# The expert jobs on TensorE: one two-way branch in place of two tests, and a prefetch hint for the narrow variant's closing jump

## The reference

```
q_n, k_n = rmsnorm(q, g_q), rmsnorm(k, g_k)            # q, k, v: 4 x 12 heads x 448 x 64
x = softmax(q_n k_n^T / 8) v                           # as rows: 1792 tokens x 768
logits = (x / |x|) (emb / |emb|)^T / tau               # 8 experts
e = argmax(logits);  gate = softmax(logits)[e]
x = gate * (relu(x @ w1[e]) @ w2[e])                   # w1[e]: 768 x 1024, w2[e]: 1024 x 768
out = (sigmoid(x @ w_gate) * (x @ w_val)) @ w_out      # 768 x 1536, 1536 x 768
```

## Time and profile before

| | us |
|---|---|
| median of three runs | 1142.76 |
| the profiled execution's own time | 1139.64 |
| span of its profile | 1138.2 |
| TensorE busy with matmuls | 1104.6 (97%) |
| TensorE weight loads | 979.2 (86%) |
| VectorE | 775.7 (68%) |
| ScalarE | 599.8 (53%) |
| GpSimd | 367.2 (32%) |

### The profile page before, as it was taken

One profiled execution on the slowest core, in us unless ns is written; L12 is line 12 of the kernel. 1 busy time (PEld: TensorE's weight loads), 2 busy tenths in 40 slices (PEclk: granted clock), 3 DMA queues, 4 the chain that ended last, 5 costly groups with the idle time before them and its releaser, 6 DMA issues. The chain is left out here.

```text
span 1138.2 us, 22080 instructions
## 1 busy us (share of the span) xinstructions
PE 1104.6 (97%) x7392; PEld 979.2 (86%) x7393; DVE 775.7 (68%) x1411; ACT 599.8 (53%) x1415; POOL 367.2 (32%) x367
## 2 busy tenths in 40 slices
PE   8999999999889899999999899999999999999997
PEld 6666666666579899999999899999999999999997
DVE  5788878997786554665466886575579675674672
ACT  5877878777536454655465752242345343441441
POOL 7798888887520110111012403000013012000002
PEclk9999999999989999999999999999999999999999
DMA  4345664444338676777687342331331434331312
GB/s 126 104 144 147 191 205 134 138 120 133 108 89 208 177 200 161 207 205 193 165 211 204 96 137 72 86 110 56 111 99 42 118 105 153 102 105 45 112 42 97
DMA packets 207778, 149.62 MB, mean 131 GB/s; under 512 B 12446, under 2 KB 203550, under 8 KB 207718
## 3 DMA queue, kind: packets, MB, share of 16 engines
q1 hardware_dynamic: 203446, 133.79, 42.3%
q0 software_dynamic: 3568, 14.82, 4.3%
q10 hardware_dynamic: 704, 0.23, 0.1%
HBM read 128.29 MB, written 20.53 MB: 131 GB/s over the span
## 5 line engine op out<-in xcount | busy, mean ns | idle before, releaser
L2059 PE MATMUL qb<-BH,l_WH 128*128 128x448 f32 x504 | 185.4, 368 | 0.6 <-DVE quads L1868 0.6
L2060 PE MATMUL qb<-BL,l_WH 128*128 128x448 f32 x504 | 185.2, 368 | 0.0
L2061 PE MATMUL qb<-BH,l_WL 128*128 128x448 f32 x504 | 185.2, 368 | 0.0
L1764 ACT ACTIVATE l_WH<-stream 128x384 fp32r<-128x384 f32 x209 | 100.7, 515 | 127.4 <-PE ob L2082 102.4
L2000 POOL TENSOR_TENSOR quads<-quads 128x448 f32<-128x448 f32 x24 | 30.7, 1278 | 381.2 <-DVE quads L1868 381.2
L1868 DVE TENSOR_TENSOR quads<-qb,quads 128x448 f32<-128x448 f32 x168 | 100.0, 619 | 67.1 <-PE qb L2061 66.9
L1864 DVE TENSOR_TENSOR l_WL<-stream,l_WH 128x384 fp32r<-128x384 f32 x209 | 121.5, 599 | 20.4 <-ACT l_WH L1764 20.3
L817 ACT ACTIVATE PR<-sc,negmax 112x448 f32<-112x448 f32 x192 | 120.7, 642 | 16.7 <-DVE negmax L535 15.9
L1605 PE MATMUL hb<-XH,W1H 128*128 128x256 f32 (+1 forms) x384 | 111.5, 290 | 5.0 <-issue 4.0
L1605 PE MATMUL yb<-HH,W2H 128*128 128x256 f32 (+1 forms) x384 | 112.9, 294 | 0.4 <-DVE W2L L1547 0.4
L2080 PE MATMUL ob<-l_WH,GH 128*128 128x384 f32 x336 | 112.5, 335 | 0.4 <-DVE Y L1948 0.4
(11 more groups left out here) (261 smaller groups left out, 2545.6 us busy)
## 6 DMA issues: line engine op xcount, KB each, us to landing
raw<-in_moe_w_dram SPq DMA_DIRECT2D x68, 384.0 KB, 5.0
stream<-in_moe_w_dram SPq DMA_DIRECT2D x48, 512.0 KB, 4.7
stream<-w_sums SPq DMA_DIRECT2D x92, 192.0 KB, 2.4
w_sums<-Sb SPq DMA_DIRECT2D x12, 768.0 KB, 6.3
stream<-in_moe_w_out_dram SPq DMA_DIRECT2D x48, 192.0 KB, 2.4
stream<-in_moe_w_val_dram SPq DMA_DIRECT2D x36, 192.0 KB, 2.7
stream<-in_moe_w_gate_dram SPq DMA_DIRECT2D x33, 192.0 KB, 2.6
raw<-in_q_dram SPq DMA_DIRECT2D x24, 224.0 KB, 3.3
```

The costliest lines, as they stand in the source:

```text
L2059: nc.tensor.matmul(bank, wh, bh, start=(k == 0), stop=False)
L2060: nc.tensor.matmul(bank, wh, bl, start=False, stop=False)
L2061: mm = nc.tensor.matmul(bank, wl, bh, start=False, stop=(k == 2))
```

## The change

The two tests become one branch with two targets, and both bodies end with a jump to a common label. For the narrow body's closing jump, a location at the body's top is marked, and the jump is tied to it by a branch prefetch hint. The wide body's closing jump has none. The work of the jobs is the same.

```diff
             with pe.Fori(0, n_jobs) as j:
                 is_long = long_job(pe, j)
-                with pe.If(is_long < 1):
+                pe.br_lt(is_long, 1, on_true="narrow_job", on_false="wide_job")
+                with nc.body("narrow_job", valid_engines=[mybir.EngineType.PE]):
+                    over_wide = pe.mark_branch_hint_location()
                     job(j, TS)
-                with pe.If(is_long > 0):
+                    pe.br("job_end").branch_hint(over_wide)
+                with nc.body("wide_job", valid_engines=[mybir.EngineType.PE]):
                     job(j, T)
+                    pe.br("job_end")
+                nc.switch_bb("job_end")
```

## The result

The changed kernel took 1134.7 us (median of ten runs, 1133.0 to 1137.33), beside 1141.78 us for the kernel before (ten runs, 1139.11 to 1145.07). The ratio is 0.9939, with a 95% interval from 0.9924 to 0.9953: 7.0 us faster (5.4 to 8.7), where 5.3 was forecast. The direction, the place and the mechanism came out as forecast; the time did not, and several of the experiments are about why.

What follows compares the result with a forecast made beforehand. TensorE, busy 97% of the span, was taken to bound the kernel. Idle gap 4.01 plus low clock 1.32 made 5.33 us, so 1142.76 - 5.33 = 1137.4 us, range 1135.0 to 1143.3.

Steps and rivals of the forecast that it cites:

- (a): Between job 0 and job 1: TensorE's idle 4.01 us goes, as the hint prefetches the closing jump's target.
- (b): Job 1's h blocks: the low clock behind the gap goes, saving 1.32 us (0.93 to 1.60).
- the sum: Whole kernel: idle gap and clock terms added, -4.01 - 1.32 = -5.33 us, all other changes taken as 0.
- The cost of the hint and of the jump: Narrow body's top and end: hint and closing jump hidden in the sequencer's lead, taken as 0 us.
- A: Job 0's closing jump: hint dropped or its block gone again, miss stays, 1142.8 us within 0.5; chance 12%.
- B: Top of job 0: the miss moves there and shows 4.62 us, time 1143.4 us; chance 7%.
- C: Later jobs: surplus hint fetches push out needed blocks, 5.33 us per miss, 1153.4 us with three; chance 6%.
- the prediction's own sign: Instruction queue 8: more packets between 376 and 640 us would mean surplus fetches by the hint.
- What the profile after would show: Instruction queue 8: the packet at 370 us would come at 333 to 345 instead.
- How the numbers follow: Final step: 1142.76 less 5.33 gives 1137.4 us, forecast 75% likely; range widened to 1135.0 to 1143.3; faster 0.70.

Runs made afterwards that it cites:

- spare body: Changed kernel plus a third, never-run body between narrow and wide; against the kernel before, ratio 1.0181 without the hint (1166.85 us), 1.0182 with it (1166.36 us).
- the test kept: Changed kernel, but the narrow body closes with the compare-and-branch of before, carrying the hint: 1135.87 us, ratio 0.9935 to the kernel before.
- the hint midway: Changed kernel with the hint marked between the narrow body's h and y blocks, 18.8 us before the first closing jump: ratio 0.9928 to the kernel before.
- both hints: Changed kernel with a second hint, on the wide body's closing jump: 1139.65 us, ratio 0.9949 to the kernel before.

## Why the prediction came out as it did, step by step

*The idle gap (a), forecast 4.01 us: right.* From the first y block of job 0 to the first h block of job 1 it takes 22.97, 23.11, 23.12 and 23.22 us in the four traces with the long closing branch and no spare body (the kernel before three times, and the one without a hint), mean 23.11. In the seven traces with an early hint (the changed kernel four times, the test kept, the hint midway, both hints) it takes 18.80 to 18.94, mean 18.85. The difference is 4.26 us. The first of the four is:

```profile
351.32:374.29 22.97, 18.96 (x164) 18.76 (x163) 10.93 (x21) 11.38 (x26) 0.00 (x0) 1.00 0.67 183
```

*The clock (b), forecast 1.32 us: right in the mean, in part by luck.* Job 1's h blocks took 18.78, 19.55, 18.82 and 19.57 us in the four, mean 19.18, and 17.62 to 18.51 in the seven, mean 17.88: 1.30 us. That the lower clock may last twice as long, 6.8 us instead of 3.4, as it did in two of the four, was not foreseen. It raises their mean 0.4 us above the 18.78 of the sum; waits for weights raise that of the seven as much above the 17.46. The two terms together are 5.56 us, where 5.33 was the sum. The expert layer as a whole says 4.6 (mean 311.3 against 306.8), with a spread of 5 us among the seven. Most of the rest is in the h blocks of jobs 3, 4, 6 and 7, which took 70.3 us together in the mean of the four traces and 71.0 in that of the seven (68.8 to 72.5). The prediction had them within 0.1 us, and no trace says that the hint is the cause.

*The cost of the hint and of the jump, forecast 0: right within what can be told.* Hint 31 to 55 ns, jump 187 ns, nearly all behind matmuls; the kernel with the test kept shows no difference. The longest branch is 0.35 us, where under 0.3 was forecast.

*The rivals.* A (the hint doesn't hold) is excluded by the trace, since the long branch is gone. B (the miss moves to the top of job 0) did not occur either: the first branch took 78 ns and the hint 55; it is what the kernel with the wide body first does. C (slower, through surplus fetches) would have been shown, by the prediction's own sign, by more packets on queue 8 between 376 and 640. They came, three of them, but with no idle time and no loss, so the sign was badly chosen and C did not occur. The Trainium skill's rule of a window of two lines ("Runtime: NRT & Kernel Launch", "Instruction fetch mechanics") does not hold for TensorE here: of six closing jumps, one missed without a hint. In the spare-body kernels its "taken branch whose target isn't in the current" window does show, four and five times, once the loop is larger.

*The packets in "What the profile after would show": wrong.* The hint at the body's top set off no packet of its own at 333 to 345; in the hinted kernel three packets stand in 333:370.5, as in the kernel before. Hinted one block ahead, a packet came at 371.1, 2.3 us behind the hint and 0.5 us before the jump began; in the kernels without a hint it came 2.2 us after the start of the long branch. What would fit is that one of the three carried the jump's target in place of the block that follows the narrow body, and that this one was fetched when the first wide job came, with two more. The trace does not say which block a packet carries, so this stays open.

*"How the numbers follow": this step failed.* It took the level from three runs (1142.76; ten gave 1141.78, so 1.0 us of the 2.7 us of error). It took the spread from them too, "some 1.9 us for a median of three runs", and 1134.7 lies further than that below 1137.4. The other 1.7 us are the size of the change, 7.1 us between the medians against 5.3: the sum put the difference in all stages that the change does not touch at nothing. The comparisons of kernels with an early hint gave gains of 7.0, 7.4, 8.2, 5.8 and 3.9 us. Most of that spread comes from outside the change. The stage ahead of the experts, whose instructions are the same in all kernels, took from 332.9 to 340.1 us in the sixteen traces, and the h blocks of jobs 3, 4, 6 and 7 together took 68.8 to 72.5 us in the changed kernel alone. The gated layer does not add to it: from its first matmul to the end it is 494.4 to 495.9 us in all sixteen. The range, drawn from one trace's terms and three runs, did not hold that.

*What remains open.* Twice the span times (1 - mean granted clock) is the time at the lower level. It was 13.2 us in the mean of the changed kernel's first ten runs. With the test kept it was 15.5, against 21.3 in the kernel before beside it, and the gain was 7.4. In the second timing of the changed kernel it was 19.6 against 19.1, and the gain was 3.9, little less than the gap alone. Within each kernel on each chip, over the 166 runs that have both numbers, a run with 1 us more at the lower level is 0.34 us longer (an estimate, by least squares; single runs scatter by 1.7 us around it). The means of the test kept, the hint midway, both hints and the second timing lie 7.3, 6.7, 5.4 and 4.0 us under the kernel before beside them; brought by that slope to equal time at the lower level, they lie 5.3, 5.3, 4.7 and 4.2 us under it. So much of the spread between 3.9 and 8.2 goes with the time at the lower level, of which the change removes only the part behind the gap. For the first comparison the clock of the kernel before is on record in one run only, so where its last 1.7 us come from stays open. Whether the change has a hand in the clock of other stages, or the chip and chance, these runs don't tell.

No experiment points to a version faster than the changed kernel; the intervals of those with an early hint overlap.

## What to carry to other kernels

A single idle gap put down to "issue" on the engine that sets the time is worth a look at its sequencer's branches: their longest against their median, and the packets of the instruction queue beside it. A jump over code that never ran cost 4.3 us of idle time and 1.3 behind it here. A hint takes it away for 31 to 55 ns; worked out from the late hints it has to stand about 5 us ahead, and the nearest that hid all of it stood 18.8 us ahead. A jump whose target was still there gained nothing from one. Before such small terms are turned into a time, the stages that the change does not touch should be looked at for their spread over executions, since here the sum from one trace was right to 0.3 us and the time still missed by 2.7.

## What the runs showed of the hardware that was not expected

- Two bodies of 1224 matmuls and weight loads together stayed in TensorE's instruction memory in the kernel before: no instruction packet came from 376 us to the end of the loop. With a third body between them, unused, the jump into the wide body and the loop's own branch behind it missed at each wide job (4.0 to 4.9 us of the sequencer, 2.9 to 4.8 us of idle TensorE).
- The granted clock fell to 0.50 in or behind all ten idle gaps of 3.75 us and more that branches left in the expert layer. With shorter ones it went either way: it fell with 1.94, 2.94 and 3.13 us, and stayed up with 1.62, 3.12 and 3.24 us.
- A taken branch that hit took 169 to 248 ns, compare-and-branch or plain jump, and now and then 312 to 390 ns, most often at the first use of a target; an untaken one took 69 to 93 ns.
